# An attention, dense-layer and eight-expert kernel: w2's scale ahead of w1's low parts, the last expert's w2 converted in one go and awaited by quarters

## The reference

```
scores = cap * tanh(scale * q @ k.T / cap); attn = softmax(scores); x = attn @ v      # 1792 x 768
y = relu(x @ w_in)**2 @ w_out                                                          # 768 -> 2048 -> 768
# routing: all (row, expert) logits in falling order; a row goes to the first expert with room
order = argsort(-(y @ w_gate).flatten()); cap = 1792 // 8
for e in range(8):
    mask = assigned == e                                   # 224 rows
    h = maximum(y[mask] @ w1[e], 0.0)                      # 768 -> 1024
    out[mask] = h @ w2[e]                                  # 1024 -> 768
```

## Time and profile before

| | us |
|---|---|
| Median of 3 runs | 1067.57 |
| Lowest and highest | 1065.84, 1069.12 |
| The profiled execution's own time | 1069.65 |
| Its span (first to last record) | 1067.9 |
| TensorE busy | 1030.7 (97%) |
| DVE busy | 804.9 (75%) |
| ACT busy | 592.3 (55%) |
| POOL busy | 196.7 (18%) |

### The profile page before, as it was taken

The page is one execution under the profiler, slowest core; times in us unless marked ns, Lnnn a source line. Parts: engine busy times, 40 slices in busy tenths (PEclk is TensorE's granted clock), DMA queues, the critical chain, the costliest instruction groups (busy, mean ns, idle before and its releaser), DMA issues.

```text
span 1067.9 us, 23597 instructions
## 1 busy us (share of the span) xinstructions
PE 1030.7 (97%) x8700; PEld 748.8 (70%) x8700; DVE 804.9 (75%) x1695; ACT 592.3 (55%) x974; POOL 196.7 (18%) x319
## 2 busy tenths in 40 slices
PE   6999999999999999999999999999996999999996
PEld 3444444444469999999976666666655999888885
DVE  4899998999968666666586667666667898888861
ACT  5888887898846333333362111313315688888891
POOL 3444444444320000000000000000001122222211
PEclk9999999999999999999999999999997999999999
DMA  3752221212024000000241040401047566677401
GB/s 93 196 151 61 60 61 50 55 52 60 18 96 151 2 2 2 2 1 2 78 161 31 16 149 16 149 16 31 16 148 260 189 249 227 249 267 287 157 14 52
DMA packets 66783, 103.45 MB, mean 97 GB/s; under 512 B 14480, under 2 KB 44432, under 8 KB 66704
## 3 DMA queue, kind: packets, MB, share of 16 engines
q1 hardware_dynamic: 64144, 91.34, 25.9%
q0 software_dynamic: 2560, 11.01, 3.4%
HBM read 91.32 MB, written 11.01 MB: 96 GB/s over the span
## 4 chain that ended last, share of the span: by engine, by line
PE 85%; DVE 7%; issue 4%; DMA 2%; ACT 1%; POOL 1%; SPq 0%; DVEq 0%; POOLq 0%; ACTq 0%
PE psum L1451 21%; PE psum L1634 17%; PE psum L1742 12%; PE psum L1728 9%; PE psum L1481 6%; PE psum L1496 5%; PE psum L1505 5%; PE psum L1637 3%; DVE arena L1028 2%; PE psum L1667 2%; PE psum L1525 2%; DMA arena<-y_rows,arena 1%; PE psum L1710 1%; PE psum L1563 1%; DVE arena L1020 1%
## 5 line engine op out<-in xcount | busy, mean ns | idle before, releaser
L1451 PE MATMUL psum<-arena 128*128 128x224 f16 x2304 | 224.3, 259 | 1.0 <-DVE arena L1000 1.0
L1451 PEld LDWEIGHTS psum<-arena 128*128 128x128 f16 x2304 | 219.7, 98 | 5.5 <-issue 2.6
L1634 PE MATMUL psum<-arena 128*128 128x384 f16 x1152 | 195.9, 326 | 0.0
L1634 PEld LDWEIGHTS psum<-arena 128*128 128x128 f16 x1152 | 107.7, 98 | 66.8 <-issue 0.8
L590 POOL TENSOR_SCALAR arena<-arena 128x448 f32<-128x448 f32 x168 | 106.0, 642 | 162.3 <-DVE arena L1010 162.3
L1742 PE MATMUL psum<-arena 128*112 128x384 f16 x768 | 127.1, 326 | 0.7 <-issue 0.7
L720 ACT ACTIVATE arena<-arena 128x448 f32<-128x448 f32 x168 | 125.9, 752 | 1.0 <-DVE arena L1030 1.0
L802 ACT ACTIVATE arena<-psum,arena 128x384 f32<-128x384 f32 x28 | 16.3, 582 | 186.5 <-PE psum L1634 144.3
L1742 PEld LDWEIGHTS psum<-arena 128*112 128x112 f16 x768 | 99.3, 130 | 25.1 <-issue 1.1
L1728 PE MATMUL psum<-arena 128*128 128x224 f16 x1152 | 113.3, 261 | 2.4 <-DVE arena L1388 2.0
L1728 PEld LDWEIGHTS psum<-arena 128*128 128x128 f16 x1152 | 111.2, 99 | 4.2 <-DVE arena L1388 2.4
(11 more groups left out here) (234 smaller groups left out, 1371.9 us busy)
## 6 DMA issues: line engine op xcount, KB each, us to landing
arena<-moe_w SPq DMA_DIRECT2D x16, 3072.0 KB, 12.1
arena<-moe_w_out SPq DMA_DIRECT2D x32, 384.0 KB, 4.2
arena<-moe_w_in SPq DMA_DIRECT2D x16, 384.0 KB, 4.6
arena<-q SPq DMA_DIRECT2D x24, 224.0 KB, 2.7
arena<-v SPq DMA_DIRECT2D x24, 192.0 KB, 2.4
arena<-k SPq DMA_DIRECT2D x24, 96.0 KB, 2.6
arena<-k SPq DMA_DIRECT2D x48, 48.0 KB, 2.3
y_rows<-arena SPq DMA_DIRECT2D x4, 336.0 KB, 2.4
```

The costliest lines, as they stand in the source:

```text
L1451: last = pe.matmul(out, w_split[:, f, z, k * 128:(k + 1) * 128], x[u % 2][:, k, :], start=(k == 0 and m == 0), stop=(k == KD - 1 and m == 2))
L1634: last = pe.matmul(psum[:, BANK_Y + q % 4, 0:HALF], g_pair(p)[:, x, k, i * 128:(i + 1) * 128], w_split[:, k, z, columns], **flags)
```

## The change

Three edits, in three engines' programs.

In DVE's step, `w2_scale(e + 1)`, four small instructions, moves from behind w1's low parts of expert e+2 to right behind the scale of the hidden rows. That holds for steps 0 to 6; in step 6 there is no expert e+2, and the order doesn't change.

In ACT's step 6, the four quarters of w2's high part of expert 7 stand together, ahead of `rows_out(1)` of expert 6; before, quarters 2 and 3 came behind it.

In TensorE's program, part 0 of the down product of expert 7 waits for w2's low quarters one after the other, each ahead of the two blocks k that read it. All other down parts wait as before.

```
@@ ACT, step @@
                 rows_out(0)
                 if is_last(e + 1):
                     eh_hi(e + 1)
-                    w2_hi(e + 1, 0, 1)
+                    w2_hi(e + 1, 0, 1, 2, 3)
                 steady = not first(e + 2) and not first(e + 1)
                 if steady:
                     w1_hi(e + 2, 0)
                     w1_hi(e + 2, 1)
                 rows_out(1)
-                if is_last(e + 1):
-                    w2_hi(e + 1, 2, 3)
@@ DVE, step @@
                     dve.tensor_tensor(o_part, eh_inv, w1_y, ALU.mult).then_inc(s_ee, 1)
                     wait(dve, s_ee, 4 * (e + 2))
+                    if not first(e + 1):
+                        w2_scale(e + 1)
                 if first(e + 1):
                     w1_lo(e + 2, 2)
...
                 if expert_live(e + 1):
-                    if not first(e + 1):
-                        w2_scale(e + 1)
                     if not is_last(e + 1):
                         rows_scale(e + 1)
@@ TensorE, expert_down(e, j) @@
                 wait(pe, s_eL, 2 * (e + 1))
-                wait(pe, s_w2L, 4 * (e + 1))
+                if j > 0 or not is_last(e):
+                    wait(pe, s_w2L, 4 * (e + 1))
                 wait(pe, s_o, 4 * e + j + 1)
...
                 for k in range(KE):
+                    if j == 0 and is_last(e) and k % 2 == 0:
+                        pe.wait_ge(s_w2L, 4 * e + k // 2 + 1)
```

## The result

The changed kernel took 1070.46 us (median of 10 runs, 1068.41 to 1071.81), the kernel before 1066.9 in the same comparison: ratio 1.0032, 95% interval 1.0022 to 1.0041, thus about 3.4 us slower. Measured a second time beside other kernels it was 1.0015 (1.0006 to 1.0024). The two intervals only just overlap, and the experiments show why one number may not be enough.

A forecast was written before the change was run, and what follows sets the result against it. The experts' stage was taken as bound by TensorE's own work, with 0.73 us to win. A 2.47 us stall less the 0.73 us gap gave +1.74 on 1067.57: 1069.3 us, range 1066.8 to 1071.4.

The forecast's parts named there:

- the likeliest case: End of the experts' stage: a stall of about 2.5 us that eats the 0.73 us gap, net +1.74 us, 1069.3 us; weight 0.79.
- the clock rival: TensorE's clock falls in the new stall, costing 1.5 us more: +3.2 us, 1070.8, up to 1071.4; chance 0.10.
- half clock in the last 26 us: Named as a sign in the profile after, at the kernel's end, that the forecast is wrong.
- the forecast's stall: TensorE waits once, about 2.5 us, between parts 2 and 3 of expert 6, for the eviction of part 1.
- Edit one, cost 0: DVE's earlier w2 scale delays low parts by 0.1 to 0.3 us in step 5, under cover; cost 0, gain 0.
- Edit two, a stall of 2.47 us: ACT's four quarters delay the eviction of expert 6's part 1, so part 3 starts at 1042.01 instead of 1039.54.
- Edit three, worth the gap alone and nothing behind the stall: Quarter waits ahead of expert 7's part 0 gain 0.73 us by themselves, nothing once the stall of edit two exists.
- The first eviction of expert 7: Waits for expert 6's scatter, ends at 1051.9; part 2 of expert 7 needs it at 1053.7: no cost.
- I think it holds the clock: The 2.47 us stall follows 25.5 us of dense matmuls, so TensorE's clock was expected to stay full.
- Half clock for 4 us: Upper end of the clock rival: half speed lasting 4 us behind the stall, time up to 1071.4.
- the price of that fall: Clock fall at about 801.5, ahead of the experts: some 3.05 us at half speed, read as costing about 1.5 us.

The follow-up runs named there:

- e1: The changed kernel with ACT's quarters 2 and 3 put back behind the eviction of part 1, early scale and quarter waits kept; 0.9996 of the kernel before.
- e10: The kernel of e1 (early scale and quarter waits, no block of four) measured again beside e9; 0.9984 of the kernel before.
- e2: The changed kernel with the wait by quarters undone, ACT's block of four and the early scale kept; 1.0019 of the kernel before.
- e5: The changed kernel as it is, measured again on one chip with other kernels; 1.0015 of the kernel before.
- e6: The changed kernel plus one ACT instruction of some 1.4 us ahead of the eviction of part 1, for a longer stall; 1.0048 of the kernel before.
- e9: The version of e8 with 9 and 2 f32 filler matmuls of 128 by 512 in place of 44 and 9 f16 ones; 0.9991 of the kernel before.
- e4: The changed kernel with three of ACT's quarters ahead of the eviction of part 1 and the fourth behind it; 1.0005 of the kernel before.
- e8: The kernel of e1 plus the filler matmuls of e7 between dense layer and experts; 0.9997 of the kernel before.
- e7: The kernel before plus 44 and 9 unread filler matmuls on TensorE where it stands still between dense layer and experts; 1.0010 of the kernel before.

## Why the prediction was right, and where it was not

The time, 1070.46, lies in the stated range, and the direction and place were right. But the likeliest case, 1069.3, was too small by half against the first measurement (+3.4 us for +1.7) and met only by the second (+1.6). What put the first inside the range was the clock rival's end, a case given 0.10. The prediction also named half clock in the last 26 us as a sign that the forecast is wrong, and that sign is there in the profile: for that execution the mechanism was the forecast's stall plus the rival's fall.

- **Edit one, cost 0.** Held: 0.17 us of delay in step 5 and 0.4 us in step 0, under cover at both places, and no wait. It was not run by itself; e1 and e10 contain it and lose nothing.
- **Edit two, a stall of 2.47 us.** Held to 0.02 us: 2.49. The low quarters ended no earlier on DVE, as worked out: 7.01 us in one piece.
- **Edit three, worth the gap alone and nothing behind the stall.** Held: 0.90 us in e1 (0.73 expected; the 0.17 us that two pieces take beyond one was left out), and 49.32 against 49.38 us with and without it.
- **The first eviction of expert 7** waits for the scatter, but not on TensorE's path: held.
- **"I think it holds the clock" failed.** I weighed a fall 2.3 us after the last matmul in rows 8 against 25.5 us of dense work ahead, and gave the clock case 0.10. The profiles of the change, e2, e5 and e6 all show the fall, 2.7, 2.4, 2.3 and 2.7 us after the last matmul; the dense work ahead gave no protection there. The rival's price of 1.5 us stood against 1.68 measured, its sum of +3.2 against 3.44 in the tail. The row was at hand; the rival should have had at least an even chance. That the second measurement came out at +1.6 is no proof of the forecast either: its profile has the fall, and its runs look like a mixture of the two cases. The rule of the Trainium skill (TensorE: Matmul & The Clock Gate, section Why this matters for your kernels) that an idle stretch amid a kernel brings the half clock back is borne out by these four profiles.
- **Two small slips.** Half clock for 4 us would cost 2.0 us and end at 1071.3, not 1071.4. And in rows 8 TensorE was at work before 812.1: twice six transposes from 807.17 on ran at half speed too, 1.38 us for six where e9's take 0.80, so that the price of that fall was more than the 1.5 us read there.

## What to carry to other kernels

When a convert or copy is moved ahead of an eviction, look up which product waits for that eviction's bank and how much it has to spare: here 0.58 us against 2.94 us. Price a new standstill of TensorE twice, once for itself and once for the clock that may fall in it. The single ones of 1.0 and 1.71 us here cost only themselves, but the pair of 1.49 and 0.91 us in attention lost the clock in half of the profiles. A mean clock over a whole execution adds up such places and doesn't tell which of them fell. And when the whole time scatters by more than the change, compare a stretch of the trace that begins behind the scatter.

## What the runs showed of the hardware

- Standstills of 1.0 us (e4) and 1.71 us (e9) kept the 2.4 GHz level; those of 2.39 us (e8), 2.49 (the change), 2.5 (e2, e5), 2.53 (e7) and 3.86 us (e6) lost it, dense work ahead or not. Each is one profile. The half speed then lasted 3.6 us after the restart in the change and 5.6 us in e6.
- Two standstills of 1.49 and 0.91 us with 0.38 us of small matmuls between them, the same in twelve profiles, lost the level in six and kept it in six, in two of the kernels differently from one execution to the next (the change and e5; e1 and e10).
- In the stretch where fillers were added, one store took 4.0 to 4.2 us to land in place of 2.5 (e7, e8, e9), in each case with an instruction load beside it.
